# Pausing GpSimd's weight split for the first low halves of u, and ending the last half batch by channel tile with three store buffers

## The chip, the cores and the metric

The kernel runs on one core of one Trainium2 chip. The metric is device time in microseconds (us). The kernel before took 945.97 us (median of three runs, 943.14 to 947.44). One more execution was taken by the hardware profiler; it took 944.42 us, and all rows in this document are from it.

## The reference, cut to what matters

Three stages follow each other: attention with a cumulative bias, a gated mixing layer, and a token and channel mixer. Only the last is touched by the change:

```python
def _moe2_ref(x, w_tok1, w_tok2, w_ch1, w_ch2):     # x: (4, 576, 512), w_ch1: (512, 1536), w_ch2: (1536, 512)
    xt = x.transpose(0, 2, 1)
    h = np.maximum(xt @ w_tok1, 0.0) @ w_tok2
    u = x + h.transpose(0, 2, 1)
    h2 = np.maximum(u @ w_ch1, 0.0) @ w_ch2
    return (u + h2).astype(np.float32)
```

## The kernel before, in words

Every fp32 product is made of three matmuls of rounded parts: each operand is held as a high part (`_hi`, rounded) and a low part (`_lo`, the rest), and `products` (L175) issues hi·hi, hi·lo and lo·hi. ScalarE usually makes the high part and VectorE the low part; of the second channel weights `c2` (called `c_hi`, `c_lo`, `c_raw` in rows, as the first ones `c1` are too) GpSimd makes both.

Attention and the gated layer fill the first part of the span, by tables of slots that set the order on each engine. The change lies behind them, in the mixer, where each of 4 batches is worked in two halves of 288 tokens (`HALF`). The channels lie in 4 tiles of 128 (`CT`), the 1536 hidden ones in 12 (`HT`). For a half batch:

- `u`: per channel tile c, VectorE adds x to the token product in PSUM and writes `u_t` (`u_sum`, L1253), ScalarE rounds it to `u_hi` (L1046), VectorE subtracts and writes `u_lo` (`u_low`, L1259). Each `u_lo` raises the semaphore `u_lo` by one. For the first half batch this runs as `start`, with nothing of the mixer before it.
- `channel(b, hf, f)`: for hidden tile f TensorE makes 12 matmuls of `u` and `c1`. At f = 0 it waits, tile by tile, for the `u_lo` of channel tile c. ScalarE (`hid_hi`, L1052) and VectorE (`hid_lo`, L1284) split the result. From f = 2 on, each call ends with the 12 matmuls of hidden tile f-2 and `c2`, three for each of four output banks `y_bank[c]`; they wait for `c2_lo` of that tile.
- `y`: once the twelfth hidden tile is in, VectorE waits for `y_filled`, which the last matmul of all four banks raises, and adds the four banks to `u_t` (L1334).
- `out`: three times (m = 0, 1, 2; 96 tokens each) TensorE transposes four tiles of `u_t` into a PSUM bank (L856), VectorE copies it to one of two halves of `o_sb` (L1280), and SyncE stores it (L516). The copy of the sixth third of a batch (m = 2 of the second half) uses the same half of `o_sb` as m = 0 did, and waits for its store to land. The transposes use the two token banks `t_bank` in turn, so m = 2 also waits for the copy of m = 0.

In the batches before the last, the channel work of the next half stands between these steps on TensorE's queue. Behind the last half batch nothing stands. GpSimd's last work in the program is the split of `c2`, 12 tiles, one copy (`c_hi`, L670) and one subtraction (`c_lo`, L673) each, straight after each other as soon as the loads are in; it begins while `start` is under way.

Of the kernel before, what the change touches and what calls it, by code (L numbers as in the profile page):

```python
# [12 lines left out]
P = 128  # L13
# [224 lines left out]
def rwkv_mixer_kernel(nc, q, k, v, s, mu_k, mu_r, w_k, w_v, w_r, w_tok1, w_tok2, w_ch1, w_ch2, out):  # L238
    with ExitStack() as ctx:
        def sem(name):  # L240
            return ctx.enter_context(nc.semaphore(name))
# [85 lines left out]
        u_hl, _ = hi_lo("k2", 1, "u", [P, CT, S])  # L327
        hid, _ = hi_lo("misc", 1, "hid", [P, 3, HALF])
        o_sb = sb("misc", 1, "o_sb", [TR, 2, DM])


        psum = ctx.enter_context(nc.psum_tensor("psum", [P, 8, BANK], F32))
# [38 lines left out]
        a_filled, a_free, u_hi, u_lo = sem("a_filled"), sem("a_free"), sem("u_hi"), sem("u_lo")  # L371
        c_filled, hid_hi, hid_lo = sem("c_filled"), sem("hid_hi"), sem("hid_lo")
        y_filled, y_added, out_stored = sem("y_filled"), sem("y_added"), sems("out_stored")

        LAST = PAIRS - 1

# [42 lines left out]
        def _(sp):  # L419
# [99 lines left out]
            with sp.Fori(0, B - 1) as b:  # L519
# [1 line left out]
                sp.wait_ge(a_free, base + FREED_X)  # L521
                load_x(b + 1)
                store(b, base, OUT_USES)
            store(B - 1, (B - 1) * USES + len(START), OUT_LAST)
            for stored_slot in out_stored:
                sp.wait_ge(stored_slot, (3 * B + 1) * 16)

# [2 lines left out]
        def _(pool):  # L530
# [136 lines left out]
            for f in range(HT):  # L667
                if f % C2_GROUP == 0:
                    pool.wait_ge(c2_in[f // C2_GROUP], C2_GROUP * 16)
                nc.gpsimd.tensor_scalar(c2[0][:, f, :], c2_raw[:, f, :], 1.0, 0.0, ALU.mult, ALU.add)\  # L670
                    .then_inc(c2_hi, 1)
                pool.wait_ge(c2_hi, f + 1)
                nc.gpsimd.tensor_tensor(c2[1][:, f, :], c2_raw[:, f, :], c2[0][:, f, :].bitcast(F32),  # L673
                                        ALU.subtract).then_inc(c2_lo, 1)
# [3 lines left out]
        def _(pe):  # L678
# [178 lines left out]
                                                   u_t[:, c, hf * HALF + n * TR:hf * HALF + (n + 1) * TR], ident[:])  # L857
                done.then_inc(a_filled, 1)

            def channel(b, hf, f):  # L860
                step = b * 2 + hf
                if f < HT:
                    if f == 0:
                        pe.wait_ge(c1_lo, len(C1_SLOTS))
                    pe.wait_ge(hid_lo, step * HT + f + 1)

                    products(nc, s_bank[f % 2][:, 0:HALF], c1, u_hl, slice(f * P, (f + 1) * P),
                             slice(hf * HALF, (hf + 1) * HALF), same(range(CT)),
                             wait=lambda c: pe.wait_ge(u_lo, step * CT + c + 1) if f == 0 else None)\
                        .then_inc(c_filled, 1)  # L870
                if f >= 2:
                    n = f - 2
                    pe.wait_ge(c2_lo, n + 1)
                    pe.wait_ge(hid_lo, step * HT + n + 3)
                    if n == 0:
                        pe.wait_ge(y_added, reach(step - 1, CT, CT))
                    for c in range(CT):
                        done = products(nc, y_bank[c], c2, hid, slice(c * P, (c + 1) * P), slice(0, HALF),
                                        [(n, n % 3)], first=n == 0, last=n == HT - 1)
                    done.then_inc(y_filled, 1)  # L880

            def mix_batch(b, with_next):
                base = b * USES + len(START)
                for kind, of_next, hf, n, nth in mixer_order(with_next):
                    if kind == "ch":
                        channel(b + of_next, hf, n)
                    elif kind != "y":
                        token(b + of_next, base, 1, kind, hf, n, nth)

# [36 lines left out]
        def _(act):  # L926
# [108 lines left out]
            def token(b, base, shift, kind, hf, n, nth):  # L1035
# [7 lines left out]
                if kind == "u":  # L1043
                    act.wait_ge(a_free, base + nth + 1)
                    cols = slice(hf * HALF, (hf + 1) * HALF)
                    nc.scalar.activation(u_hl[0][:, n, cols], u_t[:, n, cols], ACT.Copy).then_inc(u_hi, 1)  # L1046

            def hidden_hi(step, f):
                nth_hidden = step * HT + f
                act.wait_ge(c_filled, nth_hidden + 1)  # L1050
                act.wait_ge(y_filled, nth_hidden + 1)
                nc.scalar.activation(hid[0][:, f % 3, :], s_bank[f % 2][:, 0:HALF], ACT.Relu).then_inc(hid_hi, 1)  # L1052
# [30 lines left out]
            def mix_batch(b, with_next):  # L1083
                base = b * USES + len(START)
                for kind, of_next, hf, n, nth in mixer_order(with_next):
                    if kind == "ch" and n < HT:
                        hidden_hi((b + of_next) * 2 + hf, n)
                    elif kind not in ("ch", "y"):
                        token(b + of_next, base, 1, kind, hf, n, nth)

# [6 lines left out]
        def _(dve):  # L1097
# [164 lines left out]
            def token(b, base, shift, kind, hf, n, nth):  # L1262
# [13 lines left out]
                if kind == "out":  # L1276
# [2 lines left out]
                    dve.wait_ge(out_stored[o % 2], (b * 3 + o // 2 + 1) * 16)  # L1279
                    nc.vector.tensor_copy(o_sb[:, o % 2, :], bank[0:TR, :]).then_inc(a_free, 1)  # L1280

            def hidden_lo(step, f):
                dve.wait_ge(hid_hi, step * HT + f + 1)
                nc.vector.scalar_tensor_tensor(hid[1][:, f % 3, :], s_bank[f % 2][:, 0:HALF], 0.0,  # L1284
# [39 lines left out]
            def mix_batch(b, with_next):  # L1324
                base = b * USES + len(START)
                for kind, of_next, hf, n, nth in mixer_order(with_next):
                    if kind == "ch":
                        if n < HT:
                            hidden_lo((b + of_next) * 2 + hf, n)
                    elif kind == "y":  # L1330
                        dve.wait_ge(y_filled, (b * 2 + hf + 1) * HT + 3)
                        for c in range(CT):
                            cols = slice(hf * HALF, (hf + 1) * HALF)
                            nc.vector.tensor_tensor(u_t[:, c, cols], y_bank[c], u_t[:, c, cols],  # L1334
                                                    ALU.add).then_inc(y_added, 1)
# [26 lines left out]
```

## Time and profile before

| | |
|---|---|
| Median of three runs | 945.97 us (943.14 to 947.44) |
| The profiled execution: time, and its span | 944.42 us, 942.6 us |
| TensorE busy (matmuls) | 889.1 us, 94% |
| VectorE, ScalarE, GpSimd busy | 55%, 41%, 42% |
| DMA, mean rate over the span | 55 GB/s |
| The chain that ended last | TensorE 73%, GpSimd 7%, VectorE 6%, DMA 1%, SyncE's queue 1% |

The span is what the trace covers; the execution's own time is 1.8 us longer. TensorE is the engine that bounds the whole, so what counts is the few places where it stands still, and what follows its last matmul.

### The profile page before, as it was taken

The page shows a single profiled execution, that of the slowest core. Times are in us where ns is not written, and L with a number is a line of the kernel's source. Part 1 is how long each engine was busy: PE and PEld are TensorE (multiplying, and loading weights), DVE is VectorE, ACT ScalarE, POOL GpSimd, SP SyncE. Part 2 cuts the span into 40 slices and gives each one's busy share as a digit, 9 for nine tenths or more (in the row PEclk, how much of TensorE's full clock was granted, in tenths as well). Part 3 has the DMA queues.
Part 4 walks back from the last instruction along what each step waited for, and adds up shares of the span by engine and source line. Part 5 has one row for each costly group of instructions (what it writes and reads, how often), then busy time and mean ns, then how long its engine had stood idle before and what let it go on. Part 6 is the DMA issues. An engine that isn't in the chain of part 4 may idle for free.

```text
span 942.6 us, 18975 instructions
## 1 busy us (share of the span) xinstructions
PE 889.1 (94%) x6693; PEld 827.3 (88%) x6693; DVE 518.8 (55%) x1228; ACT 385.1 (41%) x985; POOL 397.0 (42%) x684
## 2 busy tenths in 40 slices
PE   5886689999999999999999999999999999999997
PEld 4665578898889988988899989999999999999996
DVE  3666767878878788687866643322323232323222
ACT  2565566566665666655634521211121112111110
POOL 4575986867777678676647418000000000000000
PEclk9997999999999999999999999999999999999999
DMA  4661212041221312202041231100010001000000
GB/s 105 198 168 39 63 40 58 27 96 39 77 64 32 96 39 63 78 27 77 2 167 43 67 108 64 51 26 1 25 50 25 0 25 50 25 0 26 1 26 26
DMA packets 79981, 51.62 MB, mean 55 GB/s; under 512 B 60320, under 2 KB 69088, under 8 KB 79904
## 3 DMA queue, kind: packets, MB, share of 16 engines
q1 hardware_dynamic: 79904, 50.63, 18.8%
q8 instruction: 44, 0.72, 0.3%
q14 instruction: 33, 0.27, 0.1%
HBM read 41.10 MB, written 9.51 MB: 54 GB/s over the span
## 4 chain that ended last, share of the span: by engine, by line
PE 73%; issue 8%; POOL 7%; DVE 6%; ACT 3%; DMA 1%; SPq 1%; DVEq 0%; POOLq 0%; ACTq 0%
PE psum L175 55%; PE psum L762 6%; PE psum L718 4%; PE psum L733 3%; POOL sq L643 2%; ACT z L946 2%; DVE z L1133 2%; POOL v_hl L566 1%; PE psum L699 1%; DVE p_t L1151 1%; POOL z L580 1%; PE psum L856 1%; POOL k_lo L647 1%; PE psum L743 1%; PE psum L836 1%
## 5 line engine op out<-in xcount | busy, mean ns | idle before, releaser
L175 PE MATMUL psum<-u_hi,c_hi 128*128 128x288 f32 x384 | 116.2, 302 | 0.9 <-DVE u_lo L1259 0.8
L1284 DVE SCALAR_TENSOR_TENSOR hid_lo<-psum,hid_hi 128x288 fp32r<-128x288 f32 x96 | 43.9, 458 | 130.8 <-ACT hid_hi L1052 130.8
L1052 ACT ACTIVATE hid_hi<-psum 128x288 fp32r<-128x288 f32 x96 | 39.5, 412 | 182.7 <-PE psum L175 182.7
L175 PE MATMUL psum<-hid_hi,c_hi 128*128 128x288 f32 x384 | 113.9, 297 | 0.0
L175 PE MATMUL psum<-hid_hi,c_lo 128*128 128x288 f32 x384 | 113.3, 295 | 0.0
L175 PE MATMUL psum<-u_hi,c_lo 128*128 128x288 f32 x384 | 113.1, 295 | 0.0
L175 PE MATMUL psum<-hid_lo,c_hi 128*128 128x288 f32 x384 | 113.1, 295 | 0.0
L175 PE MATMUL psum<-u_lo,c_hi 128*128 128x288 f32 x384 | 113.0, 294 | 0.0
L580 POOL TENSOR_SCALAR z<-cum_k,cum_qp 128x128 f32<-128x128 f32 (+4 forms) x160 | 91.9, 583 | 49.3 <-DMA cum_k<-cum_scratch 35.1
L946 ACT ACTIVATE z<-z,z_min 128x128 f32<-128x128 f32 (+4 forms) x160 | 95.1, 596 | 36.4 <-DVE z_min L1133 36.1
L1133 DVE CUSTOM_DVE_ANT_0 z<-psum,z 128x128 f32<-128x128 f32 (+4 forms) x160 | 70.5, 478 | 24.3 <-PE psum L718 18.4
L175 PE MATMUL psum<-k_hi,wv_hi 128*128 128x288 f32 x256 | 80.1, 313 | 0.0
L175 PE MATMUL psum<-xm_hi,wk_hi 128*128 128x288 f32 x256 | 79.2, 309 | 0.0
L1151 DVE TENSOR_TENSOR p_t<-psum,p_t 128x512 fp32r<-128x512 f32 (+2 forms) x112 | 66.2, 609 | 23.3 <-ACT p_t L959 20.3
L718 PE MATMUL psum<-k_t,q_t 64*64 64x288 f32 (+4 forms) x576 | 66.6, 343 | 11.4 <-DVE z_min L1133 11.2
L643 POOL TENSOR_TENSOR sq<-rel 128x288 f32<-128x288 f32 x64 | 43.5, 680 | 77.0 <-ACT k_hi L1014 76.7
L175 PE MATMUL psum<-k_lo,wv_hi 128*128 128x288 f32 x256 | 75.5, 295 | 0.0
L175 PE MATMUL psum<-xm_lo,wk_hi 128*128 128x288 f32 x256 | 75.5, 295 | 0.0
L175 PE MATMUL psum<-k_hi,wv_lo 128*128 128x288 f32 x256 | 75.5, 295 | 0.0
L175 PE MATMUL psum<-xm_hi,wk_lo 128*128 128x288 f32 x256 | 75.2, 294 | 0.0
L175 PEld LDWEIGHTS psum<-u_hi,c_hi 128*128 128x128 f32 x384 | 72.1, 188 | 3.5 <-issue 2.1
L733 PE MATMUL psum<-ident,z 128*128 128x128 f32 (+2 forms) x480 | 61.7, 269 | 13.2 <-issue 11.9
(121 smaller groups left out, 2337.9 us busy)
## 6 DMA issues: line engine op xcount, KB each, us to landing
cum_k<-cum_scratch SPq DMA_DIRECT2D x32, 288.0 KB, 3.7
q_raw<-in_q SPq DMA_DIRECT2D x32, 144.0 KB, 2.6
k_raw<-in_k SPq DMA_DIRECT2D x32, 144.0 KB, 2.8
mixed_scratch<-gate SPq DMA_DIRECT2D x32, 144.0 KB, 1.8
x_t<-mixed_scratch SPq DMA_DIRECT2D x8, 576.0 KB, 4.4
out<-o_sb SPq DMA_DIRECT2D x24, 192.0 KB, 2.1
v_raw<-in_v SPq DMA_DIRECT2D x32, 128.0 KB, 2.4
c_raw<-in_moe_w_ch SPq DMA_DIRECT2D x4, 768.0 KB, 6.5
```

The lines of the kernel that those rows point to most:

```text
L175: done = nc.tensor.matmul(out, w[a][0:r, tw, w_cols], x[b][0:r, tx, x_cols], start=first and n == 0 and m == 0, stop=last and n == len(til ...
L566: done = nc.gpsimd.tensor_tensor(v_hl[0:r, blocks, h, 1 - h, :], v_raw[0:r, blocks, h, :], v_hl[0:r, blocks, h, h, :].bitcast(F32), ALU.su ...
L580: done = nc.gpsimd.tensor_scalar(z_view(h, i), cum_k[0:r, h, 0:n], -1.0, cum_qp[0:r, i, h:h + 1], ALU.mult, ALU.add)
L643: nc.gpsimd.tensor_tensor(sq[:, f % 2, :], rel[:, f % 2, :], rel[:, f % 2, :], ALU.mult).then_inc(sq_ready, 1)
L718: done = nc.tensor.matmul(s_bank[h][0:SIZE[i], at:at + c1 - c0], q_t[hp, a, AT[i]:AT[i + 1]], k_t[hp, b, c0:c1], start=m == 0, stop=m == 2)
L733: done = nc.tensor.transpose(t_bank[bank][0:SIZE[k], n * r:(n + 1) * r], keys, ident[0:r, 0:r])
L762: done = nc.tensor.matmul(o_bank[h][:, q0:PART_W[part]], v_hl[:, b, h, :, :].rearrange("p l d -> p (l d)"), x, start=b == 0 and hl == 0, s ...
L946: nc.scalar.activation(w, w, ACT.Exp, bias=z_min[0:SIZE[i], h, i:i + 1], scale=-1.0, accum_out=z_sum[0:SIZE[i], p % 2, i, h:h + 1]).then_i ...
L1052: nc.scalar.activation(hid[0][:, f % 3, :], s_bank[f % 2][:, 0:HALF], ACT.Relu).then_inc(hid_hi, 1)
L1133: nc.vector.tensor_tensor_reduce(out=cols, in0=s_bank[h][0:r, at:at + n], in1=cols, scale=1.0, scalar=z_min[0:r, h, NBLK:NBLK + 1] if c0 e ...
L1151: nc.vector.tensor_tensor(lo, src, hi.bitcast(F32), ALU.subtract).then_inc(t_free[bank], 1)
L1284: nc.vector.scalar_tensor_tensor(hid[1][:, f % 3, :], s_bank[f % 2][:, 0:HALF], 0.0, hid[0][:, f % 3, :].bitcast(F32), ALU.max, ALU.subtra ...
```

## The change

Two edits that don't touch each other. The first: GpSimd waits, before the second of the 12 tiles of `c2`, until four low halves of `u` are written. The second: in the second half of the last batch, the last matmul of each of the banks 0 to 2 raises a new semaphore `y_end`, so that VectorE adds one bank at a time; TensorE transposes tile by tile for m = 0; the third transposed block goes to a PSUM bank that no one uses any more (`s_bank[0]`); ScalarE makes the copy of m = 1; and the copy of m = 2 goes to a third buffer `o_end`, which lies where `x_t` was.

```diff
+        o_end = sb("xm", 3, "o_end", [TR, DM])
...
+        y_end, out_filled, out_copied = sem("y_end"), sem("out_filled"), [sem(f"out_copied{i}") for i in range(3)]
...
-            store(B - 1, (B - 1) * USES + len(START), OUT_LAST)
+            store(B - 1, (B - 1) * USES + len(START), OUT_LAST[0:3])
+            for m, done in enumerate((o_sb[:, 1, :], o_sb[:, 0, :], o_end[:])):
+                sp.wait_ge(out_copied[m], 1)
+                sp.dma_start(out[B - 1, HALF + m * TR:HALF + (m + 1) * TR, :], done).then_inc(out_stored[(m + 1) % 2], 16)
...
                 if f % C2_GROUP == 0:
                     pool.wait_ge(c2_in[f // C2_GROUP], C2_GROUP * 16)
+                if f == 1:
+                    pool.wait_ge(u_lo, CT)
...
+            end_bank = [t_bank[(nth + 1) % 2] for nth in OUT_LAST[3:5]] + [s_bank[0]]
+
+            def last_out(m, nth):
+
+                if m < 2:
+                    pe.wait_ge(a_free, (B - 1) * USES + len(START) + OUT_LAST[2] + (m + 1) - 1)
+                for c in range(CT):
+                    if m == 0:
+                        pe.wait_ge(y_added, reach(2 * B - 1, CT, c + 1))
+                    at = HALF + m * TR
+                    done = nc.tensor.transpose(end_bank[m][0:TR, c * P:(c + 1) * P], u_t[:, c, at:at + TR], ident[:])
+                done.then_inc(out_filled, 1)
...
                         done = products(nc, y_bank[c], c2, hid, slice(c * P, (c + 1) * P), slice(0, HALF),
                                         [(n, n % 3)], first=n == 0, last=n == HT - 1)
+                        if end and n == HT - 1 and c < CT - 1:
+                            done.then_inc(y_end, 1)
                     done.then_inc(y_filled, 1)
...
+            def last_out():
+                act.wait_ge(out_filled, 2)
+                act.wait_ge(out_stored[0], 3 * B * 16)
+                nc.scalar.activation(o_sb[:, 0, :], t_bank[(OUT_LAST[4] + 1) % 2][0:TR, :], ACT.Copy).then_inc(out_copied[1], 1)
...
+            def last_out(m):
+                dve.wait_ge(out_filled, m + 1)
+                if m == 0:
+                    dve.wait_ge(out_stored[1], (3 * B - 1) * 16)
+                nc.vector.tensor_copy(o_sb[:, 1, :] if m == 0 else o_end[:], end_bank[m][0:TR, :])\
+                    .then_inc(out_copied[m], 1)
...
                     elif kind == "y":
-                        dve.wait_ge(y_filled, (b * 2 + hf + 1) * HT + 3)
+                        end = hf == 1 and not with_next
+                        if not end:
+                            dve.wait_ge(y_filled, (b * 2 + hf + 1) * HT + 3)
                         for c in range(CT):
+                            if end and c < CT - 1:
+                                dve.wait_ge(y_end, c + 1)
+                            elif end:
+                                dve.wait_ge(y_filled, 2 * B * HT + 3)
```

The order on GpSimd's queue where its split of `c2` begins. Before (the line numbers are those of the kernel before):

```order
L643 TENSOR_TENSOR sq<-rel 128x288 [waits k2_lo,rel_ready] x5
L670 TENSOR_SCALAR c_hi<-c_raw 128x512 [waits c2_in0]
L673 TENSOR_TENSOR c_lo<-c_raw,c_hi 128x512 [waits c2_hi]
L670 TENSOR_SCALAR c_hi<-c_raw 128x512
L673 TENSOR_TENSOR c_lo<-c_raw,c_hi 128x512 [waits c2_hi]
L670 TENSOR_SCALAR c_hi<-c_raw 128x512
```

And of the change (its own line numbers):

```order
L648 TENSOR_TENSOR sq<-rel 128x288 [waits k2_lo,rel_ready] x5
L677 TENSOR_SCALAR c_hi<-c_raw 128x512 [waits c2_in0]
L680 TENSOR_TENSOR c_lo<-c_raw,c_hi 128x512 [waits c2_hi]
L677 TENSOR_SCALAR c_hi<-c_raw 128x512 [waits u_lo]
L680 TENSOR_TENSOR c_lo<-c_raw,c_hi 128x512 [waits c2_hi]
L677 TENSOR_SCALAR c_hi<-c_raw 128x512
```

No instruction moved; the second tile's copy has a wait that it did not have, and the 21 instructions behind it on that queue stand behind the wait too.

The end of VectorE's queue, from the last hidden tiles on. Before:

```order
L1284 SCALAR_TENSOR_TENSOR hid_lo<-psum,hid_hi 128x288 [waits hid_hi] x8
L1334 TENSOR_TENSOR u_t<-psum,u_t 128x288 [waits y_filled]
L1334 TENSOR_TENSOR u_t<-psum,u_t 128x288 x3
L1280 COPY o_sb<-psum 96x512 [waits out_stored1,a_filled]
L1280 COPY o_sb<-psum 96x512 [waits out_stored0,a_filled]
L1280 COPY o_sb<-psum 96x512 [waits out_stored1,a_filled]
```

And of the change:

```order
L1325 SCALAR_TENSOR_TENSOR hid_lo<-psum,hid_hi 128x288 [waits hid_hi] x8
L1384 TENSOR_TENSOR u_t<-psum,u_t 128x288 [waits y_end] x3
L1384 TENSOR_TENSOR u_t<-psum,u_t 128x288 [waits y_filled]
L1320 COPY o_sb<-psum 96x512 [waits out_stored1,out_filled]
L1320 COPY o_end<-psum 96x512 [waits out_filled]
```

Three of the four additions no longer wait for all banks, the middle copy has gone to ScalarE's queue, and the last copy no longer waits for a store.

## Rows read from the trace of the kernel before

**Rows 1.** Windows: stretch; PE, PEld, DVE, ACT, POOL busy; PEclk, DMA share, GB/s.

```profile
646.00:880.00 234.00, 233.79 (x1723) 228.25 (x1723) 74.86 (x155) 43.34 (x97) 0.00 (x0) 1.00 0.08 23
```

**Rows 2.** Timeline of PE, 560 to 576: start, duration, instruction, [idle before <-releaser].

```profile
564.99 0.29 PE L175 MATMUL psum<-u_hi,c_hi 128*128 128x288 f32 x1
...
566.76 0.40 PE L175 MATMUL psum<-u_hi,c_hi 128*128 128x288 f32 x1 [0.81 <-DVE u_lo L1259]
...
567.54 0.40 PE L175 MATMUL psum<-u_hi,c_hi 128*128 128x288 f32 x1
...
575.16 0.29 PE L175 MATMUL psum<-hid_hi,c_hi 128*128 128x288 f32 x1
```

**Rows 3.** Timeline of DVE, 540 to 592.

```profile
563.95 0.50 DVE L1259 TENSOR_TENSOR u_lo<-u_t,u_hi 128x288 fp32r<-128x288 f32 x1
...
565.57 1.92 DVE L1259 TENSOR_TENSOR u_lo<-u_t,u_hi 128x288 fp32r<-128x288 f32 x2
568.68 0.46 DVE L1284 SCALAR_TENSOR_TENSOR hid_lo<-psum,hid_hi 128x288 fp32r<-128x288 f32 x1 [1.20 <-ACT hid_hi L1052]
...
581.87 0.88 DVE L1259 TENSOR_TENSOR u_lo<-u_t,u_hi 128x288 fp32r<-128x288 f32 x1 [0.51 <-ACT u_hi L1046]
```

**Rows 4.** Timeline of POOL, 536 to 700.

```profile
565.02 1.37 POOL L673 TENSOR_TENSOR c_lo<-c_raw,c_hi 128x512 fp32r<-128x512 f32 x1
566.35 0.83 POOL L670 TENSOR_SCALAR c_hi<-c_raw 128x512 fp32r<-128x512 f32 x1
...
585.27 1.28 POOL L673 TENSOR_TENSOR c_lo<-c_raw,c_hi 128x512 fp32r<-128x512 f32 x1
```

**Rows 5.** The tile u_lo on DVE, ns min/median/max: 562 to 568, then 600 on.

```profile
L1259 DVE TENSOR_TENSOR u_lo<-u_t,u_hi x4: 469/678/1135, 564.0 to 566.6; 128x288 fp32r<-128x288 f32 x4
...
L1259 DVE TENSOR_TENSOR u_lo<-u_t,u_hi x24: 457/459/460, 646.5 to 879.7; 128x288 fp32r<-128x288 f32 x24
```

**Rows 6.** Timeline of ACT, 540 to 592.

```profile
565.68 0.44 ACT L1046 ACTIVATE u_hi<-u_t 128x288 fp32r<-128x288 f32 x1 [0.35 <-DVE u_t L1253]
```

**Rows 7.** The chain that ended last, from 934 on: start, duration, what.

```profile
934.19 0.04 DVE u_t L1334
...
934.57 1.19 DVE u_t L1334 x3
...
935.89 0.63 PE psum L856 x4
...
937.25 2.06 DMA out<-o_sb
...
939.41 0.69 DVE o_sb L1280
```

**Rows 8.** Timeline of PE, 920 to 943.

```profile
933.45 0.30 PE L175 MATMUL psum<-hid_hi,c_lo 128*128 128x288 f32 x1
...
935.89 1.05 PE L856 MATMUL psum<-ident,u_t 128*96 128x128 f32 x8 [1.74 <-DVE u_t L1334]
```

**Rows 9.** Groups of ACT by shape: xcount | busy us, mean ns | idle before.

```profile
L1039 ACT ACTIVATE xs_hi<-psum 128x512 fp32r<-128x512 f32 x16 | 9.5, 599 | 24.0 <-PE psum L836 24.0
...
L927 ACT ACT_TABLE_LOAD x1 | 1.3, 1283 | 0.7 <-PEq L1352 0.7
```

**Rows 10.** SyncE's queue up to 939.9, then from 940; landing times of L516.

```profile
937.25 0.91 SPq L516 DMA_DIRECT2D out<-o_sb  x2
...
940.13 0.32 SPq L516 DMA_DIRECT2D out<-o_sb  x1
...
DMA to landing us min/median/max: 2.1/2.1/2.2
```

**Rows 11.** Windows around the last stores, columns as in rows 1.

```profile
937.25:937.90 0.65, 0.62 (x4) 0.39 (x4) 0.57 (x1) 0.00 (x0) 0.00 (x0) 1.00 0.00 0
...
938.40:938.90 0.50, 0.00 (x0) 0.00 (x0) 0.00 (x0) 0.00 (x0) 0.00 (x0) 1.00 0.92 299
...
939.40:939.90 0.50, 0.00 (x0) 0.00 (x0) 0.49 (x1) 0.00 (x0) 0.00 (x0) 0.80 0.15 53
```

More of the change, by code:

```diff
@@ L858, in token, with channel @@
                 done.then_inc(a_filled, 1)
-            def channel(b, hf, f):
+            end_bank = [t_bank[(nth + 1) % 2] for nth in OUT_LAST[3:5]] + [s_bank[0]]
[8 more added lines that the diff above has]
+                done.then_inc(out_filled, 1)
+            def channel(b, hf, f, end=False):
                 step = b * 2 + hf
@@ L885, in mix_batch @@
                     if kind == "ch":
-                        channel(b + of_next, hf, n)
+                        channel(b + of_next, hf, n, end=hf == 1 and not with_next)
+                    elif kind == "out" and hf == 1 and not with_next:
+                        last_out(n, nth)
                     elif kind != "y":
@@ L1087, in mix_batch @@
                         hidden_hi((b + of_next) * 2 + hf, n)
+                    elif kind == "out" and hf == 1 and not with_next:
+                        if n == 1:
+                            last_out()
                     elif kind not in ("ch", "y"):
@@ L1280, in token @@
                     nc.vector.tensor_copy(o_sb[:, o % 2, :], bank[0:TR, :]).then_inc(a_free, 1)
+            end_bank = [t_bank[(nth + 1) % 2] for nth in OUT_LAST[3:5]] + [s_bank[0]]
+            def last_out(m):
[4 more added lines that the diff above has]
+                    .then_inc(out_copied[m], 1)
             def hidden_lo(step, f):
@@ L1329, in mix_batch @@
                             hidden_lo((b + of_next) * 2 + hf, n)
+                    elif kind == "out" and hf == 1 and not with_next:
+                        if n != 1:
+                            last_out(n)
                     elif kind == "y":
-                        dve.wait_ge(y_filled, (b * 2 + hf + 1) * HT + 3)
+                        end = hf == 1 and not with_next
+                        if not end:
+                            dve.wait_ge(y_filled, (b * 2 + hf + 1) * HT + 3)
                         for c in range(CT):
+                            if end and c < CT - 1:
+                                dve.wait_ge(y_end, c + 1)
+                            elif end:
+                                dve.wait_ge(y_filled, 2 * B * HT + 3)
                             cols = slice(hf * HALF, (hf + 1) * HALF)
```

## The prediction

> **What bounds the kernel now.** I read three views in turn. The windows say where TensorE is the limit: from 646 to 880 us it is busy for 233.79 of 234.00 us at a granted clock of 1.00 (its 2.4 GHz level) [rows 1]. A gain inside that stretch would need fewer matmuls, and the change has as many as before. So only what stands before it and after it can pay: a stall of TensorE ahead of the stretch shifts everything behind it one for one, and what follows the last matmul counts in full. Then the timelines of TensorE and VectorE around the start of the channel work, where the first edit acts; then the chain that ended last, whose final pieces are the work of the second edit.
>
> **Edit 1, the pause: the stall it is aimed at.** The first `channel` call takes the four tiles of u in turn. Its first group of three matmuls starts at 564.99, the third at 566.76 after an idle of 0.81 us that a `u_lo` ended, the fourth at 567.54 [rows 2]. What is late are the third and fourth `u_lo` on VectorE, together 1.92 us from 565.57 to 567.49 [rows 3]. The same instruction of the same shape takes 457 to 460 ns in all 24 cases after 600 us, where GpSimd does nothing, but up to 1135 ns here [rows 5]. Of the four, the first took 0.50 [rows 3], the shortest 0.47 and the longest 1.14; the median of 0.68 lies between 0.50 and the one left, which is 0.86 [rows 5]. The pair is thus the third tile with 1.14 (565.57 to 566.71) and the fourth with 0.86 (566.63 to 567.49). GpSimd was in a `c_lo` from 565.02 to 566.39 and in a `c_hi` from 566.35 to 567.18 [rows 4]; each of the two `u_lo` ended 0.32 us after the GpSimd instruction under which it had started. The third tile was held as if it could not begin until GpSimd was through. A VectorE instruction that takes one operand from PSUM is not held: `hid_lo` at 568.68 ran in 0.46 us [rows 3] under GpSimd's continuing split, whose last piece ends at 586.55 [rows 4].
>
> A rule bears on this. The Trainium skill, SBUF — State Buffer, section SBUF: two separate sides, says that VectorE and GpSimd share one pair of SBUF ports under an exclusive lock, and that a VectorE instruction with two SBUF inputs stands still for the whole of a GpSimd instruction that started first. The rows above agree, with 1.14 us against 0.46. If the two merely shared bandwidth, a `u_lo` beside GpSimd would slow by a part of its length and the pause would gain less than the sum below.
>
> **Edit 1, the sum.** With GpSimd standing still from its first tile on, the third `u_lo` takes 0.46: 565.57 to 566.03. The fourth waits for its `u_hi`, 565.68 + 0.44 = 566.12 [rows 6], starts some 0.03 later and ends at 566.61. TensorE starts the group of a tile 0.04 to 0.05 after its `u_lo` (567.49 to 567.54), so the third group starts at 566.08 and the fourth at 566.65 instead of 567.54: **0.9 us**. Bounds: nothing, if the stall comes back from elsewhere; at most 1.3, which is TensorE without any wait: 234.00 us for 1723 matmuls are 0.136 each [rows 1], three groups of three 1.22, so 566.2 for the fourth. I take 0.9, since it is built from this place's own rows.
>
> What waits behind the pause: the copy of the second tile and 21 more instructions. The first tile is not held. The pause ends with the fourth `u_lo`, at 566.61. The tiles cost 2.02 us each with both instructions ((586.55 - 566.35) / 10 tiles [rows 4]), so `c_lo` of tile 1 is there at about 568.7 and of tile 11 at 588.9, some 2.3 later than before. TensorE first asks for tile 1 at 575.16 [rows 2], by then 574.3: 5.6 us of cover. After that it asks for one tile per `channel` call, and two such calls cost 24 matmuls at 0.136, 3.3 us, against GpSimd's 2.0, so the cover grows. What the later end of GpSimd's split meets are other `u_lo` (that at 581.87 is already held, 0.88 us [rows 3]); nobody waits for these before the second half batch. Cost: nothing. Without the cover it would be what tile 1 is late.
>
> **Edit 2, the end: what it removes.** I follow the chain [rows 7]. The last bank is ready and VectorE adds from 934.19, four times, until 935.76 (the last three take 1.19). Transposes run from 935.89 to 936.52, the copy of m = 0 follows, its store is issued at 937.25 and lands at 939.31; only then may m = 2 be copied, 939.41 to 940.10; its store is issued at 940.13 [rows 10].
>
> **Edit 2, the new order.** Bank 2 gets its last matmul at 933.45 + 0.30 = 933.75 [rows 8], so bank 2 is added from 933.79 to 934.25 and banks 0 and 1 before that, under TensorE's remaining products. Bank 3 is added from 934.19 as before, alone: until 934.65. Its tile is transposed 0.13 to 0.14 later (935.76 to 935.89), at 934.79; the other three tiles' transposes of m = 0 are through by then. Four transposes take 0.63 [rows 7], eight 1.05 [rows 8], so four more add 0.42, one 0.105. m = 0 is ready at 934.79 + 0.63 - 3 x 0.105 = 935.11, m = 1 at 935.53, m = 2 at 935.95, none waiting for a copy. VectorE copies m = 0 from 935.13 to 935.82 and m = 2 from 935.97 to 936.66, at 0.69 each [rows 7]. ScalarE copies m = 1; it has no row of 96x512 from PSUM, but 128x512 takes 0.60 [rows 9], so until 936.15. The bounds of that are 0.60 and, if it had to load its table again, 0.60 + 1.28 [rows 9]; since the only table load stands at the program's start and `hid_hi` and copies alternate without one, I take 0.60. SyncE issues at 935.84, 936.17 and 936.68, each 0.32 long [rows 10], so none waits for another. The last issue then moves from 940.13 to 936.68, **3.45 us** earlier.
>
> **Edit 2, what is late next: three stores at once.** A store lands 2.1 us after its issue when alone or with one beside it [rows 10], but three within 0.85 us are not in this trace. DMA is silent for about 0.65 us after an issue, then runs at 299 GB/s with two stores in flight, and is through soon after 939.40 [rows 11]: a store of 196.6 KB thus occupies the engines for 0.66 us at that rate, and 0.75 us if the two are measured from 937.9 to about 939.4. Three in a row starting at 936.5 end between 938.5 and 938.75. Alone, the third would end at about 936.68 + 0.65 + 0.75 = 938.1. So it lands 0.4 to 0.65 later than 936.68 + 2.1 = 938.78. From both sides: no delay, since landing has stayed at 2.1 to 2.2 in all shown cases, or 0.65. I take 0.4: **gain of the end 3.05 us**, ends 2.8 and 3.45.
>
> By a rule of the Trainium skill, DMA: Bandwidth & Descriptors, section Anatomy of one DMA — SWDGE (gpsimd) path, a transfer costs about 2.0 us plus its bytes at 436 GB/s, of which mostly the fixed part is waiting for the receipt. An estimate by it gives 0.45 us of moving for such a store, three would pass without queueing, and the end would gain the full 3.45. The trace's 299 GB/s is slower and decides.
>
> **Sum.** 0.9 + 3.05 = 3.95, about **4.0 us**. Against the profiled execution, 944.42 - 4.0 = 940.4. That execution lies 1.55 below the median of the three runs, so against the median: 945.97 - 4.0 = **942.0 us**, -0.42%. About 0.5%, 4.7 us, is what a measurement of this kernel can tell from no change; the runs of before themselves lie between -2.8 and +1.5 us of their median.
>
> **The rivals.**
> - *Only the end pays* (chance 0.13). The stall of the start returns under another name, the `u_hi` of the fourth tile or the PSUM additions before it. For it speaks that the fourth group needs a `u_hi` too, which is itself behind a PSUM addition (ScalarE had idled for one [rows 6]); against it that the fourth `u_lo` would need 0.9 us of other waiting, and its `u_hi` is ready at 566.12. 945.97 - 3.05 = 942.9.
> - *Both pay in full and the start a little more* (0.12). No queueing of stores (3.45) and TensorE without any wait at the start (1.3): 4.8 us, 941.2. The rows hold `u_hi` against the 1.3, so it needs ScalarE earlier as well.
> - *The third store takes the place of the wait removed* (0.05). If stores issued close together landed one behind the other at 2.06 us each, the last would land at 935.84 + 6.2 = 942.0 instead of 942.2, the end would gain 0.2, and with 0.9 the time would be 944.9. Against it: two stores were issued within 0.91 us from 937.25 [rows 10], and both were through soon after 939.4 [rows 11].
> - *Slower: the pause starves TensorE of `c2_lo`* (0.03). Place: the wait for tile 1 in the fourth `channel` call. TensorE loses what tile 1 is late beyond 574.3; tile 1 is ready 2.0 us after the pause ends. So a loss begins when the pause ends after 572.3, and eats up both gains from 576.3 on. If the count of low halves were such that the one at 581.87 ended it, tile 1 would come at 584.8, 10.5 us late: 945.97 - 4.0 + 10.5 = 952.5. Against it: four `u_lo` are issued before any channel work, and the semaphore is waited for at four.
> - *The port rule turned round*: the Trainium skill's same section lets the engine that starts first keep the port. As a mechanism of this kernel: GpSimd's longer tail would hold one more `u_lo` by up to 0.7 us (1.14 - 0.46). As nobody waits for those, it changes the time by nothing, and is counted in the forecast.
>
> **How the numbers follow.** The forecast as summed holds 0.67, its own range by the bounds of the two terms 941.2 to 943.2. Range: the other cases reach from 941.2 to 944.9; with the scatter of a median of a few runs, about 1.5 to either side, I give **939.4 to 944.8**, which leaves out some 0.15. Faster by over 0.5%: the full-gain case with 0.10 of its 0.12, and of the forecast about a fifth, where scatter adds 0.7 us, 0.14; with rounding 0.25. Slower 0.03. Within 0.5%: 0.72.
>
> **What the profile of the changed kernel would show.** Start right: the third and fourth `u_lo` at 0.46 us, GpSimd idle between its first and second tile up to about 566.6, TensorE's fourth group about 0.9 earlier, and no wait of TensorE for `c_lo`. End right: three VectorE additions before TensorE's last matmul ends, about 0.9 us from the last addition's start to the end of the first transposed block, copies of m = 0 and m = 2 back to back, three issues of SyncE within 0.9 us, and the last landing about 5.0 us (4.6 to 5.2) after the last addition begins (before: 8.0). Wrong: a landing of over 2.8 us for the third store, a table load on ScalarE ahead of its copy, a wait of TensorE for GpSimd near 574, or additions that start no earlier than before.

## The result, and the profile after

The changed kernel took 939.13 us (median of 22 runs, 936.16 to 944.41), the kernel before, run as often beside it, 944.56 (940.0 to 949.9). The ratio is 0.9944, with a 95% interval of 0.9928 to 0.996: 5.3 us less, between 3.8 and 6.8. The forecast of 4.0 us lies inside that interval; the forecast time of 942.0 does not, and its range, 939.4 to 944.8, misses the measured median by 0.3 us. The profiled execution took 937.17 us, with a span of 935.4. All ratios here compare fast runs; three runs of the experiments, of 987.76 to 1421.76 us at a granted clock of 0.84 down to 0.56, are left out.

The page of the changed kernel, its first lines and its row of the granted clock (in tenths, 40 slices):

```profile
span 935.4 us, 18972 instructions
...
PE 887.7 (95%) x6693; PEld 826.3 (88%) x6693; DVE 514.9 (55%) x1227; ACT 385.3 (41%) x986; POOL 396.5 (42%) x684
...
PEclk9996899999999999999999999999999999999999
```

VectorE's timeline where the channel work starts, which answers to [rows 3]:

```profile
557.80 0.69 DVE L1303 SCALAR_TENSOR_TENSOR h_lo<-psum,h_hi 128x512 fp32r<-128x512 f32 x1 [3.84 <-ACT h_hi L1066]
...
562.04 0.45 DVE L1291 TENSOR_TENSOR u_lo<-u_t,u_hi 128x288 fp32r<-128x288 f32 x1
562.70 0.46 DVE L1291 TENSOR_TENSOR u_lo<-u_t,u_hi 128x288 fp32r<-128x288 f32 x1 [0.22 <-ACT u_hi L1070]
564.36 0.46 DVE L1325 SCALAR_TENSOR_TENSOR hid_lo<-psum,hid_hi 128x288 fp32r<-128x288 f32 x1 [1.20 <-ACT hid_hi L1081]
```

GpSimd's, which answers to [rows 4]:

```profile
558.78 1.29 POOL L680 TENSOR_TENSOR c_lo<-c_raw,c_hi 128x512 fp32r<-128x512 f32 x1
563.25 0.62 POOL L677 TENSOR_SCALAR c_hi<-c_raw 128x512 fp32r<-128x512 f32 x1 [3.19 <-DVE u_lo L1291]
...
583.99 1.28 POOL L680 TENSOR_TENSOR c_lo<-c_raw,c_hi 128x512 fp32r<-128x512 f32 x1
```

The third and fourth `u_lo` are down from 1.14 and 0.86 to 0.45 and 0.46, GpSimd stands 3.19 us, and VectorE now waits 0.22 for the fourth `u_hi`; the prediction had this wait too, at 0.12. From the second `h_lo` to the first `hid_lo` 6.56 us pass; before it was 7.35.

The chain that ended last, from 928 us on, which answers to [rows 7]:

```profile
928.67 1.69 DVE u_t L1384 x4
930.36 0.04 issue
930.40 1.20 PE psum L877 x9
931.61 0.02 issue
931.63 0.69 DVE o_end L1320
```

SyncE's queue there, the stores' times to landing (last figure, us), and the windows over their data (columns as in rows 1), which answer to [rows 10, 11]:

```profile
931.47 0.79 SPq L529 DMA_DIRECT2D out<-o_sb  x2
932.35 0.40 SPq L529 DMA_DIRECT2D out<-o_end  x1
```

```profile
out<-o_sb SPq DMA_DIRECT2D x2, 192.0 KB, 2.2
out<-o_end SPq DMA_DIRECT2D x1, 192.0 KB, 2.6
```

```profile
932.10:932.60 0.50, 0.00 (x0) 0.00 (x0) 0.22 (x1) 0.00 (x0) 0.00 (x0) 1.00 0.65 168
932.60:933.10 0.50, 0.00 (x0) 0.00 (x0) 0.00 (x0) 0.00 (x0) 0.00 (x0) 1.00 0.89 291
933.10:933.60 0.50, 0.00 (x0) 0.00 (x0) 0.00 (x0) 0.00 (x0) 0.00 (x0) 1.00 1.00 315
933.60:934.10 0.50, 0.00 (x0) 0.00 (x0) 0.00 (x0) 0.00 (x0) 0.00 (x0) 1.00 0.96 315
934.10:934.60 0.50, 0.00 (x0) 0.00 (x0) 0.00 (x0) 0.00 (x0) 0.00 (x0) 1.00 0.27 90
```

Four additions now spread over 1.69 us, the last of them from 929.89, when the last bank is ready. From the end of the fourth addition to the first copy 0.41 us pass (930.34 to 930.75; before: 0.78, from 935.76 to 936.54). The last store is issued 2.46 us after the last bank is ready (before: 5.94) and takes 2.6 us to land instead of 2.1: the DMA engines move data for over 2 us, from about 932.1 to 934.4, at 291 to 315 GB/s in the windows that they fill. The last bank's readiness to the end of the span takes 5.48 us; before it took 8.44.

So the two stretches gained 0.79 and 2.96, 3.75 us together. But the two spans differ by 7.2. The rest stands ahead of both edits: the second `h_lo` lies at 557.80, before at 561.34, 3.54 us that no edit can have brought by its work, since GpSimd's new wait is reached only behind it and everything else later still. What could reach that far back is the changed program's layout, or chance. This is what the experiments had to settle.

### The profile page after: what moved, and what is told of

Same layout as the page of the kernel before. It is cut to its first block, busy times and chain, and to the rows that moved or that the text cites. A ratio compares the mean times of both kernels' runs of the same rounds, so it can differ in the third digit from the quotient of the medians.

```text
span 935.4 us, 18972 instructions
## 1 busy us (share of the span) xinstructions
PE 887.7 (95%) x6693; PEld 826.3 (88%) x6693; DVE 514.9 (55%) x1227; ACT 385.3 (41%) x986; POOL 396.5 (42%) x684
## 4 chain that ended last, share of the span: by engine, by line
PE 74%; issue 8%; POOL 7%; DVE 6%; ACT 4%; DMA 1%; SPq 1%; DVEq 0%; POOLq 0%; ACTq 0%
PE psum L175 56%; PE psum L769 6%; PE psum L725 3%; PE psum L740 3%; POOL sq L648 2%; ACT z L970 2%; POOL z L585 2%; POOL v_hl L571 1%; PE psum L706 1%; DVE p_t L1183 1%; DVE z L1165 1%; POOL k_lo L652 1%; PE psum L863 1%; PE psum L750 1%; PE psum L843 1%
## 5 line engine op out<-in xcount | busy, mean ns | idle before, releaser
L769 PE MATMUL psum<-p_t,v_hl 128*128 128x192 f32 (+3 forms) x448 | 70.2, 305 | 5.1 <-DVE p_t L1183 3.2
```

Source lines behind the costliest of these rows:

```text
L769: done = nc.tensor.matmul(o_bank[h][:, q0:PART_W[part]], v_hl[:, b, h, :, :].rearrange("p l d -> p (l d)"), x, start=b == 0 and hl == 0, s ...
```

## Experiments

Every kernel was profiled, and its span is cut at three moments that each kernel has: the start of the second `h_lo`, the start of the first `hid_lo`, and the moment the last bank is ready (VectorE's first addition where all four wait for it, its last where they go bank by bank). In us:

| kernel | to second h_lo | to first hid_lo | to last bank | to the end |
|---|---|---|---|---|
| before | 561.34 | 7.35 | 365.51 | 8.44 |
| changed | 557.80 | 6.56 | 365.53 | 5.48 |
| pause alone | 557.73 | 6.56 | 365.51 | 8.46 |
| end alone | 557.87 | 7.52 | 365.57 | 5.43 |
| before, with unused declarations | 564.10 | 7.96 | 365.54 | 8.45 |
| changed, second time | 563.06 | 6.56 | 365.51 | 5.48 |
| additions together | 560.83 | 6.56 | 365.51 | 6.59 |
| two store buffers | 561.04 | 6.55 | 365.53 | 6.97 |
| pause to the fifth low half | 563.05 | 6.90 | 369.34 | 5.51 |
| one store left out | 563.51 | 6.57 | 365.54 | 5.07 |
| end by column | 557.91 | 6.62 | 365.56 | 5.06 |
| changed, third time | 559.67 | 6.56 | 365.54 | 5.48 |
| before, unused declarations, second time | 560.38 | 7.32 | 365.55 | 8.45 |
| before, second time | 561.56 | 7.97 | 365.51 | 8.45 |

Four of these kernels ran once only: additions together 941.29 us, two store buffers 941.88, pause to the fifth low half 946.6, one store left out 942.48, beside 943.3 of the kernel before. Single times scatter more than these edits are worth, so only their stretches are used.

### The pause alone

Two lines of the change, in the kernel before:

```diff
+                if f == 1:
+                    pool.wait_ge(u_lo, CT)
```

> Theory A (the two edits are worth 3.7 to 3.9 us, as the stretches of the two profiles that they touch show: 0.8 at the start, 2.95 at the end; the rest of the 5.4 us between the medians is scatter of the attention stage, which the change does not touch): the pause alone gives about 0.8 us, a ratio of 0.9992, not told from 1. The third and fourth low halves of u take 0.46 us, and from the second h_lo to the first hid_lo of VectorE 6.56 us pass instead of 7.35. Theory B (some 1.5 us of the gain come with the placement of the changed program, in the stages ahead of the edits): the ratio could be as low as 0.998. Theory C (the pause is worth more than its stretch, because GpSimd meets other work later): 2 us or more, and the stretch between the first hid_lo and the last additions is shorter than 365.5 us.

Measured: ratio 1.0011 (0.9987 to 1.0036), which tells nothing about 0.8 us, though theory B's 0.998 lies just outside. The stretch tells it: 6.56, with the third and fourth `u_lo` as in the changed kernel. Behind the first `hid_lo` nothing is shorter (365.51), so theory C, a pause that pays later too, falls. VectorE there:

```profile
561.96 0.45 DVE L1261 TENSOR_TENSOR u_lo<-u_t,u_hi 128x288 fp32r<-128x288 f32 x1
562.62 0.46 DVE L1261 TENSOR_TENSOR u_lo<-u_t,u_hi 128x288 fp32r<-128x288 f32 x1 [0.21 <-ACT u_hi L1048]
```

### The end alone

The changed kernel without these lines.

> The end alone, GpSimd's split of c2 unpaused. Theory A: 2.95 us, a ratio of 0.9969; from the start of the last addition to the end of the span 5.5 us instead of 8.4, and the start as before. Theory B: 4.5 us, ratio 0.9952. Theory C: 2.95 us here and the missing 1.5 in the pause.

Measured: ratio 0.9982 (0.9954 to 1.0011): 1.7 us less, between 4.3 less and 1.0 more. Theory A's 0.9969 lies inside, theory B's 0.9952 just outside, by too little to choose by. The end took 5.43 us, the unpaused start 7.52.

### The kernel before with the change's declarations, unused

```diff
+        o_end = sb("xm", 3, "o_end", [TR, DM])
+        y_end, out_filled, out_copied = sem("y_end"), sem("out_filled"), [sem(f"out_copied{i}") for i in range(3)]
```

> The kernel before with only the declarations of the change (the buffer o_end and five more semaphores), none of them used. Theory A: ratio 1.000 within its interval. Theory B: 0.9985 or less, with the attention stage shorter by more than 1 us over several executions. Theory C: 1.000.

Measured: ratio 1.0017 (0.999 to 1.0044), so unused declarations bring no gain; theory B's 0.9985 lies outside. Its timeline of VectorE has the second `h_lo` at the latest place of all:

```profile
564.10 0.69 DVE L1273 SCALAR_TENSOR_TENSOR h_lo<-psum,h_hi 128x512 fp32r<-128x512 f32 x1 [3.84 <-ACT h_hi L1044]
```

### The changed kernel again, twice

> The changed kernel again, beside its two halves on one chip. Theory A: a ratio of 0.996 (3.8 us). Theory B: 0.9944 (5.3 us) again. Theory C: 0.9944, and more than the sum of the two halves measured alone. In its profile the stage ahead of the second h_lo again differs from that of before by some us, with the dips of the granted clock lying elsewhere.

> The changed kernel once more, to narrow its interval. If the edits are worth what their stretches show (4.1 us against the mean of the unpaused traces), 0.9957; if 5.3, 0.9944. In the trace the stretch from the second h_lo to the end of the span is 377.5 us again, and the attention stage ahead of it lies anywhere between 557 and 565 us.

Measured: 0.9945 (0.9919 to 0.997) and 0.9964 (0.9943 to 0.9985). The same program had its second `h_lo` at 557.80, 563.06 and 559.67: 5.3 us apart, more than the 4 us that its edits are worth by their stretches, while the three stretches behind it agree within 0.03 us. From the second `h_lo` on it was 377.57, 377.55 and 377.58. The first result's ratio and these two, each weighted by its width, give 0.9950 with some 0.0011 to either side: 4.7 us, 3.6 to 5.8.

The two halves, measured on the same chip as the first repeat, don't add up by their ratios: 1.0011 and 0.9982 make 0.7 us less, both together 5.2. The three intervals together allow about these 4.5 us, and by the means of the same runs the gap is 1.7 us (0.3 and 2.9 against 4.9). In the stretches there is no gap: the pause takes the start to 6.56 with or without the new end, and the new end takes 5.43 or 5.48 us with or without the pause. So nothing shows that the two edits help each other.

### The kernel before again, and its unused declarations again

> The kernel before with the change's unused declarations once more: ratio 1.000. If an unpaused start sometimes stalls TensorE long enough for its clock to fall to 1.2 GHz behind the stall, as it did behind the 2.00 us stall of the late pause, the stretch from the second h_lo to the last addition is some 1.8 us longer in one of these traces; if not, the stretch from the second h_lo to the first hid_lo lies between 7.3 and 8.0 us and the rest is 366.6.

> The kernel before, submitted as a kernel of its own, so that there is one more trace of it and a ratio of a kernel to itself: 1.000, and its distance from 1 is what this measurement can do. Second h_lo to first hid_lo 7.3 to 8.0 us, rest as in the first trace; the attention stage between 557 and 565 us, though not a line of it differs.

Measured: 0.9997 (0.997 to 1.0024) and 1.0012 (0.9986 to 1.0037). The second is the kernel before against itself: so many runs tell a ratio from 1 by a quarter of a per cent at best. No trace showed a fall of the clock behind the unpaused stall. They showed something else: the unpaused start isn't always as in [rows 3]. VectorE and GpSimd of the kernel before, second time:

```profile
564.99 1.11 DVE L1259 TENSOR_TENSOR u_lo<-u_t,u_hi 128x288 fp32r<-128x288 f32 x1
...
567.04 1.28 DVE L1259 TENSOR_TENSOR u_lo<-u_t,u_hi 128x288 fp32r<-128x288 f32 x1 [0.16 <-ACT u_hi L1046]
```

```profile
564.28 1.50 POOL L673 TENSOR_TENSOR c_lo<-c_raw,c_hi 128x512 fp32r<-128x512 f32 x1
...
566.66 1.35 POOL L673 TENSOR_TENSOR c_lo<-c_raw,c_hi 128x512 fp32r<-128x512 f32 x1
```

Here the second and the fourth `u_lo` are held, not the third and fourth, each again ending 0.31 to 0.32 us after the GpSimd instruction over it, here `c_lo` both times (565.78 and 568.01). Which tiles are held goes with the moment at which the load of `c2` lets GpSimd begin: 0.67 to 0.99 us after the second `h_lo` in the three unpaused traces with the shorter start (7.32, 7.35, 7.52), 0.00 and 0.06 in the two with the longer one (7.96, 7.97). The mean of the five is 7.62, and the pause is worth 0.76 to 1.41 us, 1.06 on the mean.

The pause leaves the first tile of the split free to run. Where its `c_hi` began 0.97 us after the second `h_lo` (end by column), the first `u_lo` started under its `c_lo` and took 0.67 us, and the start took 6.62; at 1.26 (pause to the fifth low half) they were 0.94 and 6.90.

### The end, taken apart: additions together

```diff
-                        if not end:
-                            dve.wait_ge(y_filled, (b * 2 + hf + 1) * HT + 3)
+                        dve.wait_ge(y_filled, (b * 2 + hf + 1) * HT + 3)
```

> The changed kernel, but VectorE waits for all four banks before it adds the first one, as before. If the early additions pay by taking three additions off the chain, the time from the moment the last bank is ready (first addition here, last addition in the changed kernel) to the end of the span grows from 5.5 to 6.6 us, by the 1.09 us that the last three additions start apart. If they are hidden anyway, because the transposes or the stores set the end, it stays within 0.3 of 5.5.

Measured: 6.59 us, 1.11 more, as expected. VectorE there:

```profile
932.89 1.55 DVE L1383 TENSOR_TENSOR u_t<-psum,u_t 128x288 f32<-128x288 f32 x4 [3.91 <-PE psum L175]
934.85 0.69 DVE L1320 COPY o_sb<-psum 96x512 f32<-96x512 f32 x1 [0.41 <-PE psum L877]
935.72 0.69 DVE L1320 COPY o_end<-psum 96x512 f32<-96x512 f32 x1 [0.18 <-PE psum L877]
```

From the last addition's end (934.44) to the first copy it is 0.41, as in the changed kernel: the chain is only moved by three additions.

### Two store buffers

```diff
-            for m, done in enumerate((o_sb[:, 1, :], o_sb[:, 0, :], o_end[:])):
+            for m, done in enumerate((o_sb[:, 1, :], o_sb[:, 0, :], o_sb[:, 1, :])):
...
-                if m == 0:
-                    dve.wait_ge(out_stored[1], (3 * B - 1) * 16)
-                nc.vector.tensor_copy(o_sb[:, 1, :] if m == 0 else o_end[:], end_bank[m][0:TR, :])\
+                dve.wait_ge(out_stored[1], (3 * B - (1 if m == 0 else 0)) * 16)
+                nc.vector.tensor_copy(o_sb[:, 1, :], end_bank[m][0:TR, :])\
```

> The changed kernel with two store buffers: the third block is copied to the buffer of the first, after its store has landed; additions by bank, the third PSUM bank and ScalarE's copy stay. If the third buffer removes a wait, its removal brings back 1.5 us: the last copy starts some 3.75 us after the last addition, its store is issued at 4.45, lands at 6.55, and the end comes about 7.0 us after the last addition begins, not 5.5. If three stores at once cost each other as much as the wait did, it stays near 5.5.

Measured: 6.97 us, 1.49 more. Its chain has the old wait back:

```profile
934.70 2.06 DMA out<-o_sb
...
936.86 0.69 DVE o_sb L1319
```

The additions (1.11) and the third buffer (1.49) make 2.60 of the 2.96. The last 0.36 fits the time from the end of the fourth addition to the first copy, 0.78 before and 0.41 here, since three transposes of m = 0 (0.105 each) now run ahead of that addition. No run takes this share alone, nor what the third PSUM bank and ScalarE's copy bring.

### One store left out

The store of the second block of the last half batch is not issued.

```diff
+                if m == 1:
+                    continue
...
```

> The changed kernel with the store of the second block of the last half batch left out (96 rows of the output are not written). If the third store lands late because its data queue behind the other two on the DMA engines, it now lands 2.1 to 2.2 us after its issue instead of 2.6, and the end comes 0.4 to 0.5 us earlier, 5.0 us after the last addition begins. If the 2.6 belongs to the new buffer or to its place, it stays at 2.6.

Measured: 5.07 us, 0.41 less, and the third store lands as fast as any other:

```profile
out<-o_end SPq DMA_DIRECT2D x1, 192.0 KB, 2.1
```

So the 0.5 us by which the third store of the changed kernel lands late were queueing with the other stores' data, and not the new buffer.

The prediction had set a second reckoning beside its own, by the figure of the Trainium skill, DMA: Bandwidth & Descriptors, section Anatomy of one DMA — SWDGE (gpsimd) path. Its 436 GB/s, which the page fits to DMAs issued by GpSimd, gives 0.45 us of moving for a store (an estimate), by which three would all but pass unqueued. These stores, issued by SyncE, don't bear that out: 315 GB/s was the most a window over them showed, and the third was 0.5 us late.

### The pause held to the fifth low half

```diff
-                    pool.wait_ge(u_lo, CT)
+                    pool.wait_ge(u_lo, CT + 1)
```

> The pause ends with the fifth low half of u instead of the fourth. That one is written while the fourth channel call already runs. If the cover is what the prediction said, 5.6 us and gone with this, tile 1 of c_lo comes about 2.0 us after the fifth low half and TensorE, which asks for it 6.5 us after the first hid_lo, waits some 2 us there, once; the later tiles are in time, since GpSimd makes one in 2.0 us and TensorE asks for one in 3.3 or more. The time from the first hid_lo to the last bank's addition grows from 365.5 to 367.6 us. If GpSimd had no cover or the tiles were not needed in that order, it grows by more or not at all.

Measured: TensorE does wait once for `c_lo`, 2.00 us, but the stretch grew by 3.81, to 369.34. TensorE's timeline, and the windows around it:

```profile
578.62 0.40 PE L175 MATMUL psum<-hid_hi,c_hi 128*128 128x288 f32 x1 [2.00 <-POOL c_lo L680]
...
579.71 0.44 PE L175 MATMUL psum<-hid_hi,c_hi 128*128 128x288 f32 x1
579.95 0.44 PE L175 MATMUL psum<-hid_lo,c_hi 128*128 128x288 f32 x1
```

```profile
570.00:576.00 6.00, 6.00 (x48) 6.00 (x47) 1.79 (x4) 1.25 (x3) 0.00 (x0) 1.00 0.22 76
576.00:579.00 3.00, 1.00 (x8) 0.77 (x7) 0.92 (x2) 0.43 (x2) 2.31 (x3) 1.00 0.01 3
579.00:583.00 4.00, 4.00 (x21) 4.00 (x20) 0.00 (x0) 0.00 (x0) 3.83 (x5) 0.57 0.00 0
583.00:590.00 7.00, 7.00 (x55) 7.00 (x54) 1.84 (x5) 1.27 (x3) 6.67 (x8) 1.00 0.00 0
```

The granted clock, 1.00 throughout the stall, falls behind it: 0.57 on average from 579 to 583 us, TensorE having resumed at 578.62, that is mostly at the 1.2 GHz level, with a matmul every 0.24 us instead of 0.13. The other 1.81 us are this. It is one trace; but no other of the 14 has a fall of the clock between 142 and 933 us. The start was slower as well, 6.90 for 6.56: the first `u_lo` there took 0.94 us, for it fell under tile 0 of GpSimd's split, which no pause holds.

### The end by column

The transposes of the first three channel tiles go ahead of the fourth addition; 384 columns of each token block are stored on their own, and the last 128 columns of all three blocks together.

```diff
+                if m == 2:
+                    pe.wait_ge(y_added, reach(2 * B - 1, CT, CT))
+                    for k in range(3):
+                        at = HALF + k * TR
+                        done = nc.tensor.transpose(s_bank[1][0:TR, k * P:(k + 1) * P], u_t[:, CT - 1, at:at + TR], ident[:])
+                    done.then_inc(out_filled, 1)
...
+                    sp.dma_start(out[B - 1, HALF:S, (CT - 1) * P:DM].rearrange("(m x) d -> x m d", x=TR), o_col[:])\
+                        .then_inc(out_stored[(nth + 1) % 2], 16)
```

> The changed kernel with its end cut by channel tile once more: the transposes of the first three channel tiles don't wait for the fourth; these 384 columns of the three token blocks are copied and stored on their own, and the last 128 columns of all three blocks go through one copy (VectorE) and one store; ScalarE makes two of the copies. If the end is now bound by the stores' data (590 KB at some 300 GB/s, 2.0 us, after 0.65 of silence and before 0.5 to the landing), the first issue moves from 1.58 to about 1.05 us after the last addition begins, and the last landing from 5.05 to about 4.5: the time from the last addition to the end of the span falls from 5.48 to 4.8 to 4.9. If it is bound by the last issue, that comes at some 2.2 instead of 2.46, and the gain is 0.3 or less. Or the shorter rows of the column store (512 bytes) cost more than they bring, and it is slower than the changed kernel.

Measured: 5.06 us, 0.42 less than the changed kernel; ratio to the kernel before 0.9952 (0.993 to 0.9973), median 938.37 beside 939.02 of the changed kernel on the same chip, which does not tell them apart. SyncE's queue:

```profile
931.14 0.79 SPq L537 DMA_DIRECT2D out<-o_sb  x2
931.97 0.45 SPq L533 DMA_DIRECT2D out<-o_col  x1
932.47 0.50 SPq L537 DMA_DIRECT2D out<-o_end  x1
```

The first issue comes 1.05 us after the last bank is ready (930.09), as expected for an end bound by the stores' data. But the gain was 0.42 and not the 0.6 to 0.7 that this case promised. The last issue comes at 2.38, later than the 2.2 of the other case and only 0.08 earlier than in the changed kernel, and its store lands after 2.3 us, not 2.6. The same 590 KB moved more slowly, at 241 to 277 GB/s in the windows that they fill, against 291 to 315:

```profile
932.10:932.60 0.50, 0.00 (x0) 0.00 (x0) 0.00 (x0) 0.00 (x0) 0.00 (x0) 1.00 0.94 277
932.60:933.10 0.50, 0.00 (x0) 0.00 (x0) 0.00 (x0) 0.00 (x0) 0.00 (x0) 1.00 0.85 241
933.10:933.60 0.50, 0.00 (x0) 0.00 (x0) 0.00 (x0) 0.00 (x0) 0.00 (x0) 1.00 0.97 272
```

Whether the shorter rows of these stores or their order made them slower, and which of issue and data set the end, was not tested.

## Why the prediction was wrong in its number though right in its mechanism

**Right: the start.** 0.9 us expected, 0.79 between the two profiles shown, 1.06 on the mean of all unpaused traces. The mechanism is shown by the pause alone: with GpSimd standing still each of the third and fourth `u_lo` takes 0.45 to 0.46 us, and held ones end 0.30 to 0.32 us after GpSimd's instruction in two different patterns. That agrees with the port rule that the prediction drew on (the Trainium skill, SBUF — State Buffer, section SBUF: two separate sides). What it missed is that [rows 3] is one draw of several: which `u_lo` is held varies from execution to execution.

**Right: the end.** 3.05 expected, 2.97 measured (8.45 to 5.48). The five traces with the old end took 8.44 to 8.46, the five with the new one, unaltered, 5.43 to 5.51. Term by term: the issue of the last store 3.45 earlier expected, 3.48 measured (5.94 to 2.46 after the last bank); three stores late by 0.4, measured 0.5; additions and third buffer 1.11 and 1.49, where the experiments expected 1.09 and 1.5. ScalarE's copy took 0.59 and no table was loaded.

**Right: no new wait.** No wait of TensorE for `c_lo`, and GpSimd's split ends 27.47 us after the second `h_lo` instead of 25.21, the 2.3 later that were expected; nobody waited for the later `u_lo`, of which the fifth rose to 1.00 us.

**Sum.** 3.95 expected. The stretches give 1.06 + 2.97 = 4.03 on the mean, the pooled ratio 4.7 (3.6 to 5.8). The two agree within its interval. The prediction gave 0.25 to a kernel faster by over 0.5%, which is where the first ratio, 0.9944, falls; the pooled one stands on the border.

**Wrong: the anchor.** The step that failed is "against the median: 945.97 - 4.0 = 942.0". The median of three runs stood 1.4 us above the median of 22 (944.56); from that one the same sum gives 940.6. With the same 2.6 us down and 2.8 up the range would then have been 938.0 to 943.4 and have held the measured 939.13. The text allowed 1.5 us "to either side" for the scatter of a median, as if that were a bound. The 22 runs have a standard deviation of 2.4 us, so a median of three is uncertain by some 1.6 us, one standard deviation (an estimate from them, for bell-shaped scatter). The profiled execution, 944.42, was by chance close to the true middle, and the prediction had moved away from it, to a centre that was itself one of the higher draws.

**Open: the rest.** The remaining 1.5 us, from 940.6 to 939.13, are not explained by the edits' own work. The part ahead of them scatters by 6.4 us (557.73 to 564.10) with not a line of it changed, and the kernel before with unused declarations drew the latest of them all. This scatter is nearly all made in the first 150 us. TensorE's matmuls of `xm_hi` and `wk_hi` begin between 142.2 and 148.5 us in the 14 traces, and from there to the second `h_lo` it is 414.4 to 416.8 in all of them. The first and the second trace of the changed kernel:

```profile
L175 PE MATMUL psum<-xm_hi,wk_hi x256: 288/295/402, 142.6 to 533.8; 128*128 128x288 f32 x128
```

```profile
L175 PE MATMUL psum<-xm_hi,wk_hi x256: 288/295/402, 148.5 to 539.0; 128*128 128x288 f32 x128
```

In these first 150 us lie also all falls of the granted clock but that of the late pause and those at the very end. At 90 to 110 us, before against the same kernel with unused declarations,

```profile
90.00:110.00 20.00, 13.46 (x107) 10.67 (x106) 14.81 (x36) 12.29 (x31) 17.30 (x23) 0.92 0.15 45
```

```profile
90.00:110.00 20.00, 12.14 (x75) 9.48 (x74) 14.88 (x26) 7.88 (x21) 17.10 (x24) 0.69 0.18 45
```

the granted clock was 0.92 and 0.69, and 107 matmuls began in one and 75 in the other. But the changed kernel's first trace also had 0.68 in that window, so this window alone does not order the executions. Added up, the clock stood at its lower level for some 24 us in the four traces with the fewest falls and for 34 in the two with the most, and their second `h_lo` came at 559.3 and 563.6 on the mean. The eight between overlap both, so the falls go with part of the scatter, not with all of it.

Whether the changed program's first part is truly shorter by something up to 1.5 us, or the 5.3 of the first 22 runs of each kernel was a draw from the long side, stays open. The second `h_lo` comes at 560.5 on the mean of the nine traces that have the new end, whole or altered, and at 561.0 in the other five, 0.5 us with a standard error of 1.3. That, the ratios of the repeats and those of the unused declarations speak for a draw, without excluding the other.

**The slower rival, corrected.** Its mechanism is real (the late pause), but it was priced wrongly twice. The prediction let TensorE lose what tile 1 is late and no more; a stall of 2.00 us cost 3.81, since the clock fell behind it. And the case worked out, a pause ended by the sixth low half, could not have ended at all: by the order of TensorE's queue tile 1 is asked for before the product that the sixth low half comes from. This is argued from the code; it was not run.

## What to carry to other kernels

Predict a difference by the stretches that an edit touches, and don't trust a median of three as the anchor: here it was 1.4 us off, while no term of the sum was off by more than 0.2. At the end of a kernel, count how many stores of the last block share the DMA engines: once the waits between them were gone, their queueing cost 0.4 to 0.5 us here. Where a GpSimd stream holds a short chain on VectorE that TensorE waits for, as here, try stopping it for the length of that chain, if its own product has the cover. Count what a missed cover costs with the clock's answer to the stall, here nearly as much again as the stall.

## What the runs showed of the hardware

- Behind a TensorE stall of 2.00 us at full granted clock, the clock fell to its 1.2 GHz level only after work had resumed, and cost another 1.8 us (one trace). The stalls of up to 0.82 us at the start, in all traces, had no such fall behind them.
- A VectorE instruction with two SBUF inputs that starts under a GpSimd instruction (`u_lo`, 128x288) ended 0.30 to 0.32 us after it, whether 0.16 or 0.97 us of it were left. So it took 0.47 to 1.28 us in place of 0.45 to 0.46. `hid_lo`, of the same size with one input in PSUM, took 0.46 under the same GpSimd work.
- Three stores of 196.6 KB issued within 0.88 us moved at up to 315 GB/s; the third landed after 2.6 us instead of 2.1, and after 2.1 again with one of the others left out.
